# Moving the vector steps of linear attention in a planned order of work, and splitting a small spread in four

## What is computed

```python
def phi(x):
    proj = einsum('bhsd,df->bhsf', x, w_phi)                 # 64 -> 128 features
    proj = proj - max(abs(proj), axis=-1, keepdims=True)
    return concatenate([exp(proj), exp(-proj)], axis=-1)
q_p, k_p = phi(q), phi(k)
kv = einsum('bhsf,bhsd->bhfd', k_p, v);  z = sum(k_p, axis=2)
num = einsum('bhsf,bhfd->bhsd', q_p, kv)
den = einsum('bhsf,bhf->bhs', q_p, z)[..., None] + 1e-06
x = num / den                                                # 8 heads side by side: 512 columns
xk = mu_k * x + (1 - mu_k) * x_prev;  xr = mu_r * x + (1 - mu_r) * x_prev   # x_prev: one token earlier
y = sigmoid(xr @ w_r) * (maximum(xk @ w_k, 0) ** 2 @ w_v)
```

## Time and profile before

| | |
|---|---|
| median of 3 runs | 1405.64 us (1399.19 to 1406.81) |
| the profiled execution | 1399.19 us, its span 1397.3 us |
| TensorE busy | 1331.5 us, 95% |
| VectorE busy | 756.6 us, 54% |
| ScalarE busy | 599.6 us, 43% |
| GpSimd busy | 13.1 us, 1% |

### The profile page before, as it was taken

One profiled execution on the slowest core, in us unless ns is written; L12 is line 12 of the kernel. 1 busy time (PEld: TensorE's weight loads), 2 busy tenths in 40 slices (PEclk: granted clock), 3 DMA queues, 4 the chain that ended last, 5 costly groups with the idle time before them and its releaser, 6 DMA issues. The chain is left out here.

```text
span 1397.3 us, 24914 instructions
## 1 busy us (share of the span) xinstructions
PE 1331.5 (95%) x9600; PEld 1190.0 (85%) x9600; DVE 756.6 (54%) x1275; ACT 599.6 (43%) x1079; POOL 13.1 (1%) x18
## 2 busy tenths in 40 slices
PE   6779999999999999999999999998899999999998
PEld 5648888889898888888988888998798998998997
DVE  5556545645554735554555464451855655754853
ACT  2435444454452544535435354352533433533532
POOL 0000000000000000000000000000300000000000
PEclk7679999999999999999999999999999999999999
DMA  4321202202212121220221211122110110110101
GB/s 132 111 72 50 72 16 74 74 25 71 54 53 71 40 59 31 76 65 16 76 66 36 71 50 49 56 91 48 64 65 31 42 65 31 41 64 30 41 30 38
DMA packets 92656, 78.54 MB, mean 56 GB/s; under 512 B 62736, under 2 KB 71056, under 8 KB 91536
## 3 DMA queue, kind: packets, MB, share of 16 engines
q1 hardware_dynamic: 92560, 77.09, 18.3%
HBM read 57.75 MB, written 19.02 MB: 55 GB/s over the span
## 5 line engine op out<-in xcount | busy, mean ns | idle before, releaser
L458 PE MATMUL psm<-xk_hi,wk_hi 128*128 128x288 f32 x512 | 155.4, 303 | 14.1 <-DVE xk_lo L812 5.8
L969 PE MATMUL psh<-y_hi,win_hi 128*128 128x288 f32 x512 | 154.3, 301 | 13.4 <-ACT h L1054 9.0
L817 DVE TENSOR_TENSOR k_lo<-square,k_hi 128x288 fp32r<-128x288 f32 x128 | 58.6, 457 | 197.0 <-ACT square L664 196.7
L458 PE MATMUL psm<-xk_lo,wk_hi 128*128 128x288 f32 x512 | 153.2, 299 | 0.0
L458 PE MATMUL psm<-xk_hi,wk_lo 128*128 128x288 f32 x512 | 152.8, 298 | 0.0
L970 PE MATMUL psh<-y_lo,win_hi 128*128 128x288 f32 x512 | 152.8, 298 | 0.0
L971 PE MATMUL psh<-y_hi,win_lo 128*128 128x288 f32 x512 | 152.2, 297 | 0.0
L458 PE MATMUL psm<-k_hi,wv_hi 128*128 128x288 f32 x512 | 151.8, 296 | 0.0
L458 PE MATMUL psm<-k_lo,wv_hi 128*128 128x288 f32 x512 | 151.0, 295 | 0.0
L458 PE MATMUL psm<-k_hi,wv_lo 128*128 128x288 f32 x512 | 150.8, 295 | 0.0
L1112 DVE SCALAR_TENSOR_TENSOR conv<-h,taps,conv 128x576 f32<-128x576 f32 x64 | 55.2, 863 | 142.4 <-ACT conv L1056 142.4
(11 more groups left out here) (126 smaller groups left out, 2894.7 us busy)
## 6 DMA issues: line engine op xcount, KB each, us to landing
v_nat<-in_v SPq DMA_DIRECT2D x32, 320.0 KB, 3.6
qk<-in_q SPq DMA_DIRECT2D x32, 288.0 KB, 3.1
qk<-in_k SPq DMA_DIRECT2D x32, 288.0 KB, 3.6
den<-den_scr SPq DMA_DIRECT2D x64, 144.0 KB, 2.9
y_scr<-y SPq DMA_DIRECT2D x64, 144.0 KB, 2.0
y<-y_scr SPq DMA_DIRECT2D x8, 1152.0 KB, 5.4
out<-rows SPq DMA_DIRECT2D x32, 256.0 KB, 2.0
stage<-in_moe_w_in SPq DMA_DIRECT2D x4, 512.0 KB, 3.3
```

Of the source, the lines that this page charges most:

```text
L458: return nc.tensor.matmul(o, lhsT, rhs, start=first, stop=last, skip_group_check=True)
L817: nc.vector.tensor_tensor(k2_lo[:, i, :], square[:, i % 2, :], k2_hi[:, i, :].bitcast(F32), ALU.subtract).then_inc(k2_lo_ready, 1)
L969: nc.tensor.matmul(o, wh, xh, start=first, stop=False, skip_group_check=True)
```

## The change

Four edits:
1. The planner: the tiles that were placed half behind E and half behind QT all stand behind E; RC is due 3.8 instead of 2.5 us of planned time behind NUM, DV 9.5 instead of 8.5.
2. The opening's list: NUM of pair p-1 stands ahead of EK and QT of pair p instead of behind them, and the weight pieces stand behind M, KV and NUM instead of EK, KV and NUM.
3. `spread_den` issues four transfers of one row to 64 partitions each, instead of two of two rows to 128 partitions.
4. `divide` no longer waits for the mixes that still read x.

```diff
-FILL_NS = {"E": 1600, "QT": 1600, "EK": 3200, "PICK": 3200, "NUM": 1600}
-FIRST_FILL, RC_AFTER, DV_AFTER = 4000, 2500, 8500
+FILL_NS = {"E": 3200, "EK": 3200, "PICK": 3200, "NUM": 1600}
+FIRST_FILL, RC_AFTER, DV_AFTER = 4000, 3800, 9500
@@ first_attention_steps
-    steps = []
+    steps = [("E", 0)]
     for p in range(PAIRS):
-
-        def before(*names):
-            return [(s, p - 1) for s in names] if p else []
-
-        steps += [("E", p), ("QT", p), ("EK", p)] + before("DEN", "NUM") + before("RC")
-        steps += [("M", p), ("KV", p), ("PICK", p)] + before("DV")
-    p = PAIRS - 1
-    steps += [("DEN", p), ("NUM", p), ("XK", 2, 0), ("HK", 2, 0), ("LK", 2, 0), ("RC", p)]
-    steps += [("XR", 2, 0), ("HR", 2, 0), ("LR", 2, 0), ("DV", p)]
+        last = p == PAIRS - 1
+
+        def before(s):
+            return [(s, p - 1)] if p else []
+
+        steps += [("EK", p), ("QT", p)] + before("RC") + [("M", p), ("KV", p), ("PICK", p)] + before("DV")
+        steps += [] if last else [("E", p + 1)]
+        steps += [("DEN", p), ("NUM", p)]
+        if last:
+            steps += [("XK", 2, 0), ("HK", 2, 0), ("LK", 2, 0), ("RC", p)]
+            steps += [("XR", 2, 0), ("HR", 2, 0), ("LR", 2, 0), ("DV", p)]
@@ spread_den
-            for e in range(2):
-                sp.dma_start(den_parts[:, e, :], den_rows[32 * e:32 * e + D + 1:D, :]).then_inc(den_spread, 16)
+            for h in range(2):
+                for e in range(2):
+                    row = 32 * (2 * h + e)
+                    sp.dma_start(den_parts[D * h:D * h + D, e, :], den_rows[row:row + 1, :]).then_inc(den_spread, 16)
@@ the work of SP, ScalarE and VectorE, each
-                if m is None and kind in ("EK", "KV", "NUM") and pieces < len(PIECES):
+                if m is None and kind in ("M", "KV", "NUM") and pieces < len(PIECES):
@@ copy_den and invert: den_spread counts 64 instead of 32 per pair
@@ divide
-            await_(dve, r_mixed, 2 * XT, a, 0)
```

More of the change, by code:

```diff
@@ L647, in copy_den @@
             await_(act, attended, PAIRS, a, p + 1)
-            await_(act, den_spread, 32 * PAIRS, a, 32 * p)
+            await_(act, den_spread, 64 * PAIRS, a, 64 * p)
             nc.scalar.activation(den_rows[:], q_cols(1, p, a), ACT.Copy).then_inc(den_copied, 1)
@@ L772, in invert @@
         def invert(p, a):
-            await_(dve, den_spread, 32 * PAIRS, a, 32 * (p + 1))
+            await_(dve, den_spread, 64 * PAIRS, a, 64 * (p + 1))
             await_(dve, inverse_stored, 16 * PAIRS, a, 16 * p)
```

## The result

| | median | range | ratio to before, with its 95% interval |
|---|---|---|---|
| before | 1406.22 us | 1399.19 to 1407.47 | |
| after | 1475.38 us | 1469.95 to 1480.54 | 1.0505 (1.0466 to 1.0545) |

The change makes the kernel 5% slower: +69 us at the medians, where +37 against the profiled execution was forecast and 1456 us was the upper end of the range. The profiled execution took 1474.48 us, its span is 1472.6, against 1397.3: 75.3 us more.

The account below looks back on a forecast made before the run. A chain of engine hand-offs was taken to bound the opening, TensorE the loop. Loop +23.4, opening +13 and spread +0.5 gave 36.9 us, 1436 from the profiled 1399.2; with half the median's 6.4 excess, 1439 us, range 1412 to 1456.

Parts of the forecast that it names:

- QT0 behind K04: Each loop pass, first pair: QT waits for tile K04's low half, so M0 comes 1.57 us later.
- QT1 behind XR10: Each loop pass, p=1: three mixes go ahead of QT1, so M1 comes 1.1 us later.
- QT3 behind K15: Each loop pass, p=3: QT waits for tile K15's low half, so M3 comes 1.6 us later.
- the second pair: Each loop pass, p=2: the same work stands in front of QT2, so the cost is 0.
- the waits for `max_blocks`: Loop, before PICK at p=1 and p=3: TensorE's 14 waits go, giving back 6.5 us.
- the gaps of 6.47 (6.5): Opening, pairs 1 to 3: NUM to M takes 6.5 us instead of 2.66, +3.8 each, +11.4 together.
- the waits given back: Opening: the waits for `max_blocks` of 2.5 and 1.0 us go, because RC comes early beside a later M: -3.5.
- pair 3's KV at the lower clock: Opening: behind a 6.5 us gap two groups of KV matmuls run at the low clock, +4.1 us.
- the two reasons given for the end of the `max_blocks` waits: Loop: PICK comes after KV, now over a microsecond later, and M is no longer behind DV.
- The spread: Opening's end: four transfers of den add two issues on SP, set at +0.5 us, bounds -1.0 and +1.15.
- the sum of the loop: Seven passes: 4.27 us a pass of late M, 29.9, less 6.5 of removed waits, gives +23.4 us.
- Rival 2: Loop: the clock falls behind the new gaps too, 1.7 us each, 24 more if all 14 did, 1460 us; chance 0.08.

Follow-up runs that it names:

- fill_only: The kernel before with FILL_NS alone of the planner's edit, RC_AFTER and DV_AFTER as before: 1460.71 us, 1.0418.
- due_only: The kernel before with RC_AFTER and DV_AFTER alone of the planner's edit, FILL_NS as before: 1394.95 us, 0.9932.
- planner_busy: planner_only plus 31 repeated matmuls a pass, filling TensorE's gaps before M0, M1 and M3, result unchanged: 1420.71 us, 1.0134 of before.
- gap kernels: planner_busy with the repeats before M0 left out, those before M1 left out, or about half of each: 1469.65, 1445.34, 1446.55 us.
- same_count kernels: planner_busy with repeats moved behind M0, M1, M3, or half of each moved, instead of left out: 1452.21, 1434.93, 1443.47, 1446.69 us.
- planner_only: The kernel before with the planner's edit alone (FILL_NS, RC_AFTER, DV_AFTER): 1467.22 us, 1.0445.

## Why the prediction was wrong

**What held.** Each added wait came out as worked out: QT0 behind K04 1.6 to 1.7 (forecast 1.57), QT1 behind XR10 0.86 (1.1), QT3 behind K15 1.61 (1.6), the second pair nothing; 29.1 us in all (29.9), and the waits for `max_blocks` gone. Idle time in the passes rose by 22.2, forecast 23.4. In the opening, the gaps of 6.47 (6.5), the waits given back, pair 3's KV at the lower clock: 14.0 with the spread, forecast 13.5. That these agree to half a microsecond is partly luck, since unchanged openings differ by up to 4.8 us; the gaps in it are what was forecast rightly. Of the two reasons given for the end of the `max_blocks` waits each is enough by itself: they are gone in fill_only, where M stays behind DV, and in due_only, where KV comes hardly later. The wait taken out of `divide` was not tried by itself.

**The spread** was set at +0.5 and measured +1.13 (3.70 - 2.57), its upper bound. The added issues are paid nearly in full and the transfer gained next to nothing by its new form. Of the two rules of the Trainium skill's page "DMA: Bandwidth & Descriptors" that I weighed, the one against splitting over partition halves agrees with the trace. The other's number of engines does too: the traces have 256 packets of 36 bytes for either form, and beside them 4 of 4 bytes for the old one and 64 for the new, that is 2 and 16 for each transfer. But the 36-byte packets follow each other no faster, at most 30 in 0.1 us before and 26 after, so the quicker transfer that I drew from this rule isn't there.

**The step that failed** is the sum of the loop, "29.9 - 6.5 = +23.4 us", which counts idle time only and leaves the clock at 1.00. The runs showed a mean grant of 0.95 in the passes, below the 0.98 that the prediction gave as a sign of being wrong, and 40.1 us more of busy time; planner_busy, where TensorE isn't idle in these places, has a grant of 1.00 and doesn't pay them. Rival 2 named it, with a chance of 0.08, and two of its readings were at fault. First, the chance: "the mean of the loop is 1.00, so such stretches are rare there" reads a loop that had next to no idle gap in front of KV; it says nothing of a loop with three. Its own row, 1.93 us idle and then a grant of 0.66, was the longest of five gaps at the heads of the passes in the same trace (1.33 to 1.93 us), and the clock fell behind it alone. None of the five stands in front of KV. I took "a little shorter" as a reason against, and for the heads it would have been one; in front of KV gaps of 1.6 to 1.7 us were followed by a fall 34 of 63 times. Second, the price: 1.7 us came from the earlier trace rows, a stretch with K tiles behind it. In front of KV a fall lasted 10.2 us in most cases, three times as long, and cost 5.1. Nine stretches (and the end of a tenth) cost 40 us, more than the "all 14" of rival 2 at 24.

For the opening I had expected just this (a gap in front of KV, and KV cold) and priced it; the same rule was not carried into the passes.

**What stays open.** Why the clock fell behind one gap and not behind the next of the same length and surroundings, and more often behind M0 than M3; whether KV's short matmuls are what sets its gaps apart from those at the heads; and what the second stall at the head of a pass in the three gap kernels is. It is there with a part of the 31 added matmuls in the loop, and not with all or none of them. The profile pages count 81 or 82 packets of 16 KB on the queue that loads instructions in the gap kernels and 77 in planner_busy and the same_count kernels, but before and after have 81 without a second stall, so this isn't shown as the cause.

## What to carry to other kernels

Where TensorE runs saturated at the full clock, an idle gap costs its own length and may cost a fall of the clock behind it, here above all in front of a run of short matmuls: 22 us more of idle time cost 40 more of busy time. So ask of each moved step not only how late it comes, but whether TensorE has matmuls to do meanwhile, and what follows the gap. Work placed in front of the waiting matmul can be worth more than its time; here this was tried with repeated matmuls, not with a tile moved there. And take a bundle of planner edits apart: the two due times by themselves gain 0.7%, and beside the new FILL_NS nothing of it is to be seen.

## What the runs showed of the hardware that was not expected

- Added matmuls made a kernel faster: 217 repeats in the gaps, 46 us less at the medians than the idle gaps, 44 by the ratios (planner_busy 1420.71, 1.0134; planner_only 1467.22, 1.0445).
- Gaps of 1.6 to 1.7 us in front of KV were followed by a fall in 34 of 63 cases, and gaps of 0.8 to 0.9 us before M0 and M3 in 7 of 28. Of twelve gaps of 1.60 to 1.75 us in front of a K tile none was, and where it fell behind a longer one there, it was for 3.4 us and not for 10.2.
- Leaving out 12, 7 or 16 of the 31 added matmuls gave a second stall of 1.0 to 3.0 us at the head of five of the seven passes; moving them instead did not.
